# Counts of four columns a product, 224-row last groups, and a later load for the second expert

## The reference

```python
X = np.fft.fft(np.fft.fft(x, axis=1), axis=2).real        # x: 4 x 2496 x 256

# first mixture of experts: a balanced assignment by sorted logits
for idx in np.argsort(-(x @ w_gate).flatten()):
    tok, e = idx // 8, idx % 8
    if assigned[tok] >= 0 or counts[e] >= 1248: continue
    assigned[tok] = e; counts[e] += 1
out[assigned == e] = relu(x[assigned == e] @ w1[e]) @ w2[e]     # 256 -> 1024 -> 256

# second mixture: by the largest logit, with no limit
e_idx = argmax(x @ w_gate)
out = softmax_weight * sigmoid(x @ w_output_gate)[e_idx] * (relu(x @ w1[e_idx]) @ w2[e_idx])
```

## Time and profile before

| | |
|---|---|
| median of 3 runs | 1402.94 us (1402.28 to 1404.41) |
| the profiled execution | 1403.07 us, with a span of 1401.3 us |
| granted TensorE clock, mean | 0.924 |
| busy | TensorE 1293.0 us (92%), its weight loads 1195.6, VectorE 750.0, GpSimd 561.6, ScalarE 329.3 |
| stages, by the page's slices and the timeline | to about 155 us Fourier part; to 307 assignment; 307 to 862 stage 1; from 876 stage 2 |

### The profile page before, as it was taken

One profiled execution on the slowest core, in us unless ns is written; L12 is line 12 of the kernel. 1 busy time (PEld: TensorE's weight loads), 2 busy tenths in 40 slices (PEclk: granted clock), 3 DMA queues, 4 the chain that ended last, 5 costly groups with the idle time before them and its releaser, 6 DMA issues.

```text
span 1401.3 us, 31585 instructions
## 1 busy us (share of the span) xinstructions
PE 1293.0 (92%) x10842; PEld 1195.6 (85%) x10843; DVE 750.0 (54%) x1978; ACT 329.3 (23%) x796; POOL 561.6 (40%) x548
## 2 busy tenths in 40 slices
PE   5999899829999999999999996999999999999996
PEld 4757788717988898888999986999999999999996
DVE  2733788885657568876554454433443344333442
ACT  0103110022322223232333331222222222222221
POOL 2800002314456374747556553331444142444411
PEclk9999755558999999999999998899999999999998
DMA  9605441011212122222232212221223122232110
GB/s 344 230 4 181 174 152 62 32 51 48 91 39 68 61 68 71 69 69 70 70 98 79 77 56 77 70 75 45 68 73 105 41 72 72 75 103 72 45 42 20
DMA packets 70735, 116.25 MB, mean 83 GB/s; under 512 B 7785, under 2 KB 50546, under 8 KB 70641
## 3 DMA queue, kind: packets, MB, share of 16 engines
q1 hardware_dynamic: 46864, 72.36, 15.4%
q0 software_dynamic: 11808, 31.03, 6.7%
q10 hardware_dynamic: 11968, 11.63, 3.0%
HBM read 81.83 MB, written 34.45 MB: 83 GB/s over the span
## 4 chain that ended last, share of the span: by engine, by line
PE 75%; DVE 9%; issue 2%; DMA 1%; ACT 1%; POOL 0%; ACTq 0%; POOLq 0%; DVEq 0%; SPq 0%
PE bank L1053 22%; PE bank L1055 21%; PE bank L1054 21%; PE bank L963 4%; PE bank L946 2%; DVE hot_r L1681 2%; PE bank L1192 1%; PE bank L1065 1%; DVE hot_q L1682 1%; DVE hot_q L1680 1%; DVE arena L1571 1%; DMA arena<-spectrum,idxe 0%; DVE hT_low L1848 0%; DVE xT_low L1841 0%; DVE arena L1565 0%
## 5 line engine op out<-in xcount | busy, mean ns | idle before, releaser
L1053 PE MATMUL bank<-weights_high,hT_high 128*128 (+1 forms) x1328 | 388.4, 292 | 0.0
L1055 PE MATMUL bank<-weights_high,hT_low 128*128 (+1 forms) x1328 | 378.3, 285 | 0.0
L1054 PE MATMUL bank<-weights_low,hT_high 128*128 (+1 forms) x1328 | 377.0, 284 | 0.0
L1053 PE MATMUL bank<-xT_high,weights_high 128*128 128x256 f32 (+1 forms) x1072 | 337.7, 315 | 7.5 <-DVE xT_low L1841 4.1
L1055 PE MATMUL bank<-xT_high,weights_low 128*128 128x256 f32 (+1 forms) x1072 | 333.9, 311 | 0.0
L1054 PE MATMUL bank<-xT_low,weights_high 128*128 128x256 f32 (+1 forms) x1072 | 333.4, 311 | 0.0
L1054 PEld LDWEIGHTS bank<-weights_low,hT_high 128*128 128x128 f32 x1328 | 250.5, 189 | 0.0
L1053 PEld LDWEIGHTS bank<-weights_high,hT_high 128*128 128x128 f32 x1328 | 250.2, 188 | 0.1
L1055 PEld LDWEIGHTS bank<-weights_high,hT_low 128*128 128x128 f32 x1328 | 250.2, 188 | 0.0
L1053 PEld LDWEIGHTS bank<-xT_high,weights_high 128*128 128x128 f32 x1072 | 206.0, 192 | 21.6 <-DVE xT_low L1841 4.9
L1055 PEld LDWEIGHTS bank<-xT_high,weights_low 128*128 128x128 f32 x1072 | 204.9, 191 | 11.8
(11 more groups left out here) (249 smaller groups left out, 1459.4 us busy)
## 6 DMA issues: line engine op xcount, KB each, us to landing
arena<-middle ACTq DMA_DIRECT2D x44, 258.0 KB
spectrum<-arena SPq DMA_DIRECT2D x39, 256.0 KB, 2.2
arena<-in_w2a_t SPq DMA_DIRECT2D x8, 1024.0 KB, 4.9
raw<-in_w1a SPq DMA_DIRECT2D x8, 1024.0 KB
raw<-in_w2a SPq DMA_DIRECT2D x8, 1024.0 KB
raw<-in_w1b SPq DMA_DIRECT2D x8, 1024.0 KB
raw<-in_w2b SPq DMA_DIRECT2D x8, 1024.0 KB
arena<-in_x SPq DMA_DIRECT2D x4, 768.0 KB, 4.8
```

The costliest lines, as they stand in the source:

```text
L1053: pe.matmul(out_, a[0], b[0], start=start, stop=False)
L1054: pe.matmul(out_, a[0], b[1], start=False, stop=False)
L1055: return pe.matmul(out_, a[1], b[0], start=False, stop=stop)
```

## The change

**Counts.** For phases 5 and 6 `above_count` gives way to `above_quads`: four columns of `above` (4 x 32 values) are the weights of one product, and the same four columns of `hot8` (4 x 8) move, so the result is 128 x 32, of which only the four 32 x 8 blocks on the diagonal are wanted. A rest of two columns goes first in its piece. VectorE's `spread_quads` multiplies by a mask `own` that keeps these blocks; TensorE's `fold_quads` adds the four groups of 32 rows with one f32 product against `fold`; VectorE's `mark_folded` adds the four blocks of columns and compares. `FOLD_BEHIND = 6` places the fold behind chunk 6 and the compare behind the seventh `h_out`. The pieces of `compare` are 24, 28 and 26 columns in place of three of 26.

**Groups of two tiles** are `ROWS = 224` wide in `hidden` and both `h_out`s.

**The way in.** `expert_of` for slots 1 to 4 goes behind `h_out` 1 to 4 of the first group, and SP waits for the fourth gather before it reads slot 1.

```diff
@@ -63,11 +63,13 @@
 CLOSE_AT = {3: 5, 7: 6}
 FINAL_AT = 7
 COUNT_BEHIND = {-1: 3, 3: 3, 7: 3}
-MARK_BEHIND = 4
+MARK_BEHIND, FOLD_BEHIND = 4, 6
 PROBES = 32
 ROUNDS = 4
 CHUNKS = (0, 24, 48, 68, N // P)
-LATER_CHUNKS = (0, 26, 52, N // P)
+LATER_CHUNKS = (0, 24, 52, N // P)
+QUAD = 4
+assert QUAD * PROBES == P
 DCH = D // P
 FCH = F // P
 
@@ -79,6 +81,7 @@
 FIRSTS = list(range(0, TPE, GT))
 TILES = [min(GT, TPE - k) for k in FIRSTS]
 NG = len(FIRSTS)
+ROWS = [min(w * P, CAP - k * P) for k, w in zip(FIRSTS, TILES)]
 SPLITS = 8
 PW = (DCH * F + FCH * D) // SPLITS
 LG = 2 * E
@@ -165,6 +168,8 @@
     parts = (np.arange(PROBES) + 1) * float(PROBES) ** -(np.arange(ROUNDS)[:, None] + 1)
     put("parts", np.append(parts.reshape(-1), 0.0)[None, :])
     put("lane2", p + P)
+    put("own", p // PROBES == np.arange(QUAD * E)[None, :] // E)
+    put("fold", p % PROBES == np.arange(PROBES)[None, :])
     put("valid", (np.arange(TPE) * P + p < CAP))
     put("beyond", 16.0 * E * REG * (np.arange(TPE) * P + p >= CAP))
     return cos_n, sin_n, c
@@ -468,8 +475,14 @@
             before = min(ph, SERIAL) * ROUNDS * (len(CHUNKS) - 1) + max(ph - SERIAL, 0) * ROUNDS * (len(LATER_CHUNKS) - 1)
             return before + r * (len(chunks(ph)) - 1)
 
-        def count_at(ph):
-            return bank[0][0:PROBES, 0:E] if ph < SERIAL else bank[7][0:PROBES, 64:64 + E]
+        def count_at():
+            return bank[0][0:PROBES, 0:E]
+
+        def quads_at():
+            return bank[7][:, 384:384 + QUAD * E]
+
+        def folded_at():
+            return bank[7][0:PROBES, 416:416 + QUAD * E]
 
         def move_at(ph):
             return bank[1][:, 0:E] if ph < SERIAL else bank[7][:, 80:80 + E]
@@ -610,6 +623,7 @@
             weights(m1, 0, expert_of(0), w1a, w2a)
             for e in range(4, E):
                 turned_weights(e)
+            sp.wait_ge(m1.got[GT - 1], 16)
             for slot in range(1, E):
                 weights(m1, slot, expert_of(slot), w1a, w2a)
             for e in range(2):
@@ -956,12 +970,30 @@
 
             def above_count(ph, r):
 
-                to, pieces = count_at(ph), chunks(ph)
+                to, pieces = count_at(), chunks(ph)
                 for c in range(len(pieces) - 1):
                     pe.wait_ge(s_above, above_done(ph, r) + c + 1)
                     for j in range(pieces[c], pieces[c + 1]):
                         mm = pe.matmul(to, above[:, j, :], hot8[:, j, :], start=(j == 0), stop=(j == NT1 - 1))
                 mm.then_inc(s_above_ps, 1)
+
+            def above_quads(ph, r):
+
+                to, pieces = quads_at(), chunks(ph)
+                for c in range(len(pieces) - 1):
+                    pe.wait_ge(s_above, above_done(ph, r) + c + 1)
+                    j, odd = pieces[c], (pieces[c + 1] - pieces[c]) % QUAD
+                    while j < pieces[c + 1]:
+                        w = odd if j == pieces[c] and odd else QUAD
+                        mm = pe.matmul(to[0:w * PROBES, 0:w * E], above[:, j:j + w, :].rearrange("p j k -> p (j k)"),
+                                       hot8[:, j:j + w, :].rearrange("p j e -> p (j e)"), start=(j == 0), stop=(j + w == NT1))
+                        j += w
+                mm.then_inc(s_above_ps, 1)
+
+            def fold_quads(ph, r):
+
+                pe.wait_ge(s_spread, (ph - SERIAL) * ROUNDS + r + 1)
+                pe.matmul(folded_at(), cc("fold"), spread[:], start=True, stop=True).then_inc(s_folded, 1)
 
             def move(ph, r):
 
@@ -1038,12 +1070,16 @@
 
             def route_count(G, f):
 
+                if f == FOLD_BEHIND and G in COMPARE_AT:
+                    ph, r = COMPARE_AT[G]
+                    route_read(s_pass, ph * ROUNDS + r + 1)
+                    fold_quads(ph, r)
                 if f != COUNT_BEHIND.get(G, 1):
                     return
                 if G in COMPARE_AT:
                     ph, r = COMPARE_AT[G]
-                    route_read(s_pass, ph * ROUNDS + r + 1)
-                    above_count(ph, r)
+                    route_read(s_spread, (ph - SERIAL) * ROUNDS + r + 1)
+                    above_quads(ph, r)
                 if G == FINAL_AT:
                     route_read(s_closed, E - SERIAL)
                     new_count(E - 1, hot8)
@@ -1069,7 +1105,7 @@
                 def hidden(e, s, gi, f):
 
                     n = e * (NG * FCH) + (gi * FCH + f)
-                    w = TILES[gi] * P
+                    w = ROWS[gi]
                     if f == 0:
                         pe.wait_ge(m.xT, e * TPE + (FIRSTS[gi] + TILES[gi] + 2))
                         if gi == 0:
@@ -1574,7 +1610,18 @@
             def mark(ph, r):
 
                 dve.wait_ge(s_above_ps, ph * ROUNDS + r + 1)
-                dve.tensor_tensor(passes[:], count_at(ph), left_open[0:PROBES, :], ALU.is_ge).then_inc(s_pass, 1)
+                dve.tensor_tensor(passes[:], count_at(), left_open[0:PROBES, :], ALU.is_ge).then_inc(s_pass, 1)
+
+            def spread_quads(ph, r):
+
+                dve.wait_ge(s_above_ps, ph * ROUNDS + r + 1)
+                dve.tensor_tensor(spread[:], quads_at(), cc("own"), ALU.mult).then_inc(s_spread, 1)
+
+            def mark_folded(link, ph, r):
+
+                dve.wait_ge(s_folded, (ph - SERIAL) * ROUNDS + r + 1)
+                link(dve.tensor_reduce(counts[:], folded_at().rearrange("p (j e) -> p e j", e=E), AX.X, ALU.add))
+                dve.tensor_tensor(passes[:], counts[:], left_open[0:PROBES, :], ALU.is_ge).then_inc(s_pass, 1)
 
             def table(ph, r):
 
@@ -1749,8 +1796,6 @@
             dve.wait_ge(s_hot_used, BATCHES)
             rows(link, bank[2][:, 0:2 * q].rearrange("p (o q) -> p o q", o=2), *LISTS[0])
             dve.sem_inc(m1.row, 1)
-            for slot in range(1, SERIAL):
-                expert_of(link, slot)
 
             on_limit = Count(dve, s_limit)
 
@@ -1827,9 +1872,14 @@
             def marking(G):
 
                 if G in COMPARE_AT:
-                    mark(*COMPARE_AT[G])
+                    spread_quads(*COMPARE_AT[G])
                 if G == FINAL_AT:
                     counted_new(on_limit.link, E - 1)
+
+            def folded(G):
+
+                if G in COMPARE_AT:
+                    mark_folded(on_limit.link, *COMPARE_AT[G])
 
             def stage1(m, fast):
 
@@ -1927,6 +1977,8 @@
                                 h_out(*nxt, f)
                                 if fast and f == MARK_BEHIND:
                                     marking(e * NG + gi)
+                                if fast and f == FOLD_BEHIND:
+                                    folded(e * NG + gi)
                             gated(e, gi)
                             h_out(*nxt, 7)
                         else:
@@ -1949,6 +2001,10 @@
                 h_out(0, 0, f)
                 if f == MARK_BEHIND:
                     marking(-1)
+                if f == FOLD_BEHIND:
+                    folded(-1)
+                if 1 <= f < SERIAL:
+                    expert_of(on_limit.link, f)
             for e in range(E):
                 expert(e, e % 2, e == E - 1)
```

## The result

The kernel after the change takes **1381.61 us** (median of 4 runs, 1380.75 to 1382.42) against 1402.61 us for the kernel before (the three runs above and a fourth, 1401.39 to 1404.41): ratio **0.9848**, with a 95% interval of 0.9836 to 0.986. The forecast was 1380.8. The profiled execution took 1381.85 us, with a span of 1380.0; that of the kernel before had 1401.3.

A forecast was written before the change was run, and what follows sets the result against it. TensorE, busy 1293 of 1401.3 us, was taken as the bound. From 1403.07 us, -3.1 (way in) - 8.9 (counts) - 11.4 (gaps) + 2.4 (added wait) - 1.3 (224 columns) gave 1380.8 us, range 1371 to 1393.

The forecast's parts named there:

- The way in: Start of stage 1: the second expert's load no longer holds up the gathers, first product 3.1 us earlier.
- A count: TensorE's counts fall from 2.24 to 0.97 us, fold of 0.25 included; seven of eight gain, 8.9 us.
- The wait at `places`: TensorE stands before `places` for the later compare, about 0.3 us in seven counts: 2.4 us lost.
- The gaps: Issue gaps in the counts of groups 2 and 5, and the lower clock behind, go: 11.4 us gained.
- 224 columns: 384 products of the short groups narrow from 256 columns, down to a weight floor of 115 ns: 1.3 us gained.
- The rival where the gaps stay: Gaps in groups 2 and 5 remain, so 11.4 us less is gained: 1392.2 us, chance 0.10.
- The slow gathers: Rival at the way in: gathers are slow at their own pace, load or not: 1383.9 us, chance 0.07.
- the slower rates under 256 columns: Rivals: 224-column products run at the four-pass f32 rate, 1481 us, chance 0.08, or two-pass, near no change, 0.03.

The follow-up runs named there:

- the second set: Runs on another chip: the changed kernel again against the kernel before (1389.28 us) took 1378.70 us, ratio 0.9925.
- the first pair: The first profiled traces of the kernel before and the changed kernel, from the comparison of 1402.61 with 1381.61 us.
- 156 products: Kernel before with the counts of groups 1, 3 and 4 done twice in a row: 1409.58 us against 1403.91.
- one moved group: Kernel before with the four scatters of expert 0 alone moved one expert later: 1385.53 us against 1390.08.
- widths: Changed kernel with last-group products 256 to 64 columns wide, by expert: 118.4 ns a product at 256, 109.9 at 64.

## Why the forecast was right, and where it was not

The total was right: 21.9 us gained by the end of stage 1 against 22.3 forecast, 21.0 in the medians. Part of this is luck. Single terms were off by up to 1.5 us in both directions and cancel, and the comparison fell into a set of runs that has the gaps; in the second set the same change gained 10.6. Its steps:

- **The way in**, -3.1: -3.44 measured, of which 0.26 was there before the gathers began. The mechanism holds, with one part idle: SP's wait.
- **A count**, 2.24 to 0.97: it went to 0.80 and a fold of 0.38, so 1.18. Two sizes were off. The price of 26 ns for a product of 128 weight columns was right (25 ns measured), but the odd product of two columns was priced like the others and costs 0.20 us more. And the fold costs 0.38 with its breaks (from the chunk before it to the one behind it, 396.03 to 396.87, less two steps), not 0.25. Over seven counts that is 7.4 in place of 8.9.
- **The wait at `places`**, +2.4: 0.17 us in the five groups with wide products and 0.35 in the two short ones, 1.55 in all. The mechanism and the order (short ones worse) were right; the two operations take 0.36 us with their hand-over (397.69 to 398.05), about as supposed. With the counts the net is -5.9 against -6.5, and the counts alone gave 6.3.
- **The gaps**, -11.4: in the first pair the old kernel's groups 2 and 5 are 5.84 and 5.68 us longer than in the second set, 11.5 together, so the size was read rightly. The new form removed them, but in their place ScalarE's late relu costs 0.73 and 0.78 us in the same two groups, which the forecast did not have; 10.0 net. The cause that it named, a supply that "this dense run uses up", is wrong as it stands: 156 products pass without a gap, so a dense run alone does not do it. What does is open (below). It also took the gaps for a property of the kernel. They are one of the chip or the set, and in a set without them this term is 0. Nor does the lower clock need a gap, as the single runs of the 224 rows and of 156 products showed.
- **224 columns**, -1.3: -2.1. Six short groups without a count give 0.14 to 0.29 us each, 1.5 together; the other two are put at 0.3 each, an estimate. The floor is right; it lies at 111 ns and not at 115.

Added up: 3.4 + 5.9 + 10.0 + 2.1 = 21.4. Of the 0.5 that are left of the 21.9, 0.4 is the short break in the old count of group 6. The rival where the gaps stay would have left a gain of 10.9 us. In the second set the gain is 10.6, but not by its mechanism: there neither kernel has gaps. The slow gathers, and the slower rates under 256 columns, did not come.

The changed kernel itself differs between the sets by 2.9 us in the medians (1381.6 and 1378.7), and by 3.6 us at the end of stage 1 in the two traces. 1.5 of the 3.6 are the two late relus. The rest, 1.9 us, is group 12, whose step is 27.2 us in ten of the fourteen traces and 25.3 in four (old and new counts, three of the sets among them); no edit here goes with the one or the other.

**What stays open:** why TensorE gets four products and then nothing for 0.5 us, in groups 2 and 5 and in some sets only. For the four scatters speak the times (the gap begins 1.7 to 1.8 us behind the start of the first and ends 0.9 to 1.0 us behind the end of the last, not 1.5 us as the expectation for one moved group has it) and that ScalarE is late in the same stretch when TensorE is not. Four scatters of group 1 beside dense products of 125 ns bring nothing, but this does not speak against a supply that they slow. An estimate from the trace of the kernel before: some 14 products pass in the gap, the 4.15 us from 394.66, so 0.3 us each. Group 1's scatters stand from 366.9 to 373.5, if 2 us behind the last start are counted as in group 2. At that rate 22 products would come in these 6.6 us where 53 are used. The 31 that are short are fewer than the 46 that pass ahead of a gap. The kernels that would tell, with the scatters moved and the counts kept, were run only where there were no gaps. The page also lists 57 packets of 16 KB in a queue of kind "instruction", in both kinds of set. The Trainium skill, "Runtime: NRT & Kernel Launch", section on instruction fetch, says that blocks of that size are fetched ahead and that crossing one is "mostly hidden". No run here shows what a crossing costs, and the packets do not stand at one place beside the gaps. In the kernel before one passes at 400.1 us, behind the end of the first gap, and one at 474.3, inside the second. In the run with 156 products they pass at 393.4 and 410.5, on either side of the first gap.

## What to carry to other kernels

Before a gap that no row explains is put into a forecast, profile the same kernel in another set of runs, best on another chip: about half of the 21 us here hung on gaps that three of five sets did not have. In a row of equal small products, price the odd one apart: one product of another shape made up 0.2 of the 0.7 us of a count. And where a result is made later to save work, look for the engine that stands before it at every place: moving the compare one chunk earlier only changed who waited.

## What the runs showed of the hardware

- The same kernel takes about 1390 us in three sets of runs and 1403 in two. In two of its traces, one of each kind, each instruction of stage 1 starts at the same time within 0.1 us up to the count of group 2. Most of the difference (11.5 us) is two stretches of 4 us with few products, and half the clock for about 4 us behind each.
- The granted clock also fell to 0.5 for 3.4 us behind rows of small products without a gap: behind 78 of 8 columns (379.4 us, only 224 rows), behind 156 (381.0 and 439.1, doubled counts), and behind 48 of 64 columns (833.6, widths). Behind most counts of 78 it did not fall.
- TensorE's products of type fp32r with 128 weight columns step at 110 to 112 ns at the seven widths tried from 64 to 240, 118 at 256 and 232 at 512.
- 128 bf16 weight columns with 32 moving step at 25 ns, 32 with 8 moving at 25 to 26 ns. One product with 64 weight columns among those with 128 makes the row 0.20 us longer.
- The profile writes down the added 0.17 us before `places` as "issue" on the weight load; only the distance from the last product shows it. The 0.35 us of the short groups are listed, as two waits for `passes` of 0.2.
